# A linear-attention, routed-expert and gated-layer kernel: the attention stage laid out over 128 partitions, two batches at a time, with loads on two queues

## Chip, core and metric

The kernel runs on one core of a Trainium2 chip. Its five engines are TensorE (PE in the profile, its weight loads apart as PEld), VectorE (DVE), ScalarE (ACT), GpSimd (POOL) and SyncE (SP). The metric is the device time of one execution, in microseconds (us); lower is better.

## What is computed

Three layers follow each other. The first one, attention without a softmax, is where most of the change lies.

```python
def _attn_ref(q, k, v, g_norm):                  # each 8 x 8 x 576 x 64 (batch, head, token, width)
    kv = np.einsum('bhsd,bhse->bhde', k, v)
    out = np.einsum('bhsd,bhde->bhse', q, kv)
    rms = np.sqrt(np.mean(out * out, axis=-1, keepdims=True) + 1e-06)
    return (out / rms * g_norm)

def _moe_ref(x, modality_id, w_gate, modality_bias, w1, w2):   # x: 4608 x 512, 8 experts, F = 1024
    logits = x @ w_gate + modality_bias[modality_id]
    e_idx = np.argmax(logits, axis=1)
    ...
    for e in range(E):
        mask = e_idx == e
        h = np.maximum(x[mask] @ w1[e], 0.0)
        out[mask] = gate_w[mask, None] * (h @ w2[e])

def _moe2_ref(x, w_gate, w_val, w_out):           # 512 -> 1536 -> 512
    gate = 1.0 / (1.0 + np.exp(-(x @ w_gate)))
    val = x @ w_val
    return (gate * val @ w_out)
```

All inputs are float32.

## The kernel before

The program has four stages: attention, routing, expert tiles, gated layer. Each engine runs its own stream of instructions, and the streams meet only in semaphores (`wait_ge`, `then_inc`).

**Attention.** A batch's 576 tokens lie on R = 96 partitions, J = 6 tokens on each. So one partition's run in a load of q, k or v is 6 x 64 floats, 1536 bytes for each head, and a batch's load of one of the three is 1152 KB. SyncE issues all loads, one queue, double-buffered by batch (L384, L385, L387). One *step* handles one of the six tokens of each partition, for all eight heads, so there are 48 steps (8 batches of 6). Work of different steps overlaps: `At(i, s, lag)` says which step an operation serves. In a step

- ScalarE gathers the step's q out of `qt` into `qp` (L550); TensorE transposes it, four transposes (L926); ScalarE copies the result to `qT` (L530);
- TensorE multiplies `qT` by `kvx`, four matmuls (L911), one per pair of heads. `kvx` holds, for each pair, the two 64 x 64 products of k and v and 16 further columns, which are those products times the router's weights, so the router's logits come out of the same matmul. The outputs stand in one of two places in PSUM (`pair_outs`), so the matmuls of step n wait for the last reader of step n - 2 (`lgh_made`);
- ScalarE squares (L517), VectorE sums (L714), ScalarE takes the root (L512), VectorE the reciprocal (L692), VectorE normalises the outputs into `xn` (L704) and the router's columns into `lgh` (L708), and adds these up over heads into `logits` (L696) a step later;
- GpSimd multiplies `xn` by `g_norm` into `xb` (L457). SyncE stores `xb` to HBM once a batch is complete.

In four of the six steps TensorE also computes the k-v products of the batch, 12 matmuls of 96 rows by 64 columns a step (L942). In the other two it makes the router's columns: ScalarE copies the products to `kvx` (L539), TensorE transposes (L950), ScalarE copies to `kvT` (L544), TensorE multiplies by the router's weights (L918), ScalarE copies (L524). These chores are spread over the steps.

During attention, SyncE also loads the first expert's eight weight units (512 KB each, into the two buffers `raw`), behind the batches' loads, and VectorE splits them in each step into a high and a low part (L673, L679), since the expert matmuls work with float32r high parts and low remainders.

**Routing.** Once all logits are there, VectorE picks experts, counts and makes one-hot tables (L728 to L773, most on arrays of 96 x 384). 48 matmuls, one per step column, turn these into the token tables (L962), which VectorE reads (L784). GpSimd then gathers the first tile of tokens (L477).

**Experts and gated layer.** Tiles of 128 tokens, gathered by expert, pass two matmuls each; the next expert's weights are loaded into `raw` and split by VectorE meanwhile. Then come nine blocks of 512 tokens through the gated layer, bound by TensorE (L1047, L1058).

## Time and profile before

| | us |
|---|---|
| median of 3 runs | 1633.44 |
| fastest, slowest run | 1631.88, 1639.65 |
| span of the profiled execution | 1628.0 |
| TensorE busy in that span | 1547.1 (95%) |
| mean granted TensorE clock | 0.978 of full |

The profile gives the profiled execution its span, from first to last instruction; what a timed run has around the span is the difference, 5.4 us to the median. A granted clock of 1.00 in the rows is 2.4 GHz, 0.50 is 1.2 GHz. "DMA share" is how busy the core's 16 DMA engines were on average; it can read a little over 1 since a packet's record spans its overlap with the next.

### The profile page before, as it was taken

The numbers are of one execution on the slowest core, as the hardware profiler recorded it, in microseconds if no ns is written. First come the engines' busy times: TensorE is split into PE (matmuls) and PEld (weight loads), VectorE is DVE, ScalarE is ACT, GpSimd is POOL, SyncE is SP. The second block draws the span as 40 slices with busy tenths as digits, with TensorE's granted clock in tenths as the row PEclk, the third lists the DMA queues.
The fourth block names the chain that finished last, engine by engine and source line by source line (L and its number), as shares of the span: only waits on it lengthen the run. The fifth ranks groups of instructions, "written<-read, shape, count | busy, mean of one in ns | idle before, by whom it ended". The sixth has DMA issues, their size and how long they took to land.

```text
span 1628.0 us, 23019 instructions
## 1 busy us (share of the span) xinstructions
PE 1547.1 (95%) x7924; PEld 1297.4 (80%) x7925; DVE 559.8 (34%) x938; ACT 397.9 (24%) x744; POOL 181.3 (11%) x298
## 2 busy tenths in 40 slices
PE   6988479999999999969999999999999999999998
PEld 5878368888888888858888888888888888888886
DVE  2877743364524552233312212122121221212111
ACT  2766112222222222233221211112111121111111
POOL 1443122222222222100000000000000000000000
PEclk9999589999999999989999999999999999999999
DMA  9998223243314332043110000101001010010000
GB/s 226 257 266 232 81 75 106 71 154 129 120 47 136 112 128 64 31 134 103 65 52 1 30 23 1 53 1 52 1 1 52 1 52 1 0 52 0 27 0 26
DMA packets 56321, 120.61 MB, mean 74 GB/s; under 512 B 7614, under 2 KB 32190, under 8 KB 55488
## 3 DMA queue, kind: packets, MB, share of 16 engines
q1 hardware_dynamic: 49856, 99.75, 20.9%
q0 software_dynamic: 6400, 19.93, 4.0%
q8 instruction: 49, 0.80, 0.2%
q14 instruction: 16, 0.13, 0.0%
HBM read 91.33 MB, written 29.38 MB: 74 GB/s over the span
## 4 chain that ended last, share of the span: by engine, by line
PE 58%; issue 25%; DMA 6%; POOL 4%; POOLq 3%; DVE 1%; SPq 1%; ACT 0%; DVEq 0%; ACTq 0%
PE ps L1047 36%; PE ps L1058 18%; DMA vt<-in_v 4%; POOL xg L477 3%; POOLq L476 2%; PE ps L942 1%; PE ps L911 1%; PE ps L1037 1%; DMA raw<-in_moe_w 1%; POOL hold L471 1%; POOL from_now L475 1%; POOLq L484 0%; DMA x_rows<-xb 0%; DVE ssum L714 0%; POOL y_rows L485 0%
## 5 line engine op out<-in xcount | busy, mean ns | idle before, releaser
L1047 PE MATMUL ps<-yhi,gv 128*128 128x512 f32 x1728 | 548.1, 389 | 1.5 <-DVE ylo L874 1.5
L1047 PEld LDWEIGHTS ps<-yhi,gv 128*128 128x128 f32 x1728 | 324.3, 188 | 69.2 <-issue 1.9
L1047 PE MATMUL ps<-ylo,gv 128*128 128x512 f32 x864 | 336.1, 389 | 0.0
L1058 PE MATMUL ps<-wo,shi 128*128 128x512 f32 x864 | 266.9, 390 | 1.4 <-DVE slo L892 1.4
L890 DVE TENSOR_TENSOR s<-ps,sig 128x512 f32<-128x512 f32 x108 | 74.7, 692 | 489.2 <-ACT sig L609 489.2
L992 PE MATMUL ps<-ew,xhi 128*128 x640 | 203.3, 399 | 2.2 <-DVE xlo L811 1.7
L1014 PE MATMUL ps<-ew,hhi 128*128 x640 | 197.2, 389 | 1.3 <-DVE hlo L822 1.3
L1058 PEld LDWEIGHTS ps<-wo,shi 128*128 128x128 f32 x864 | 161.5, 188 | 35.0 <-DVE slo L892 1.9
L1047 PEld LDWEIGHTS ps<-ylo,gv 128*128 128x128 f32 x864 | 162.2, 188 | 33.7
L609 ACT ACTIVATE sig<-ps 128x512 f32<-128x512 f32 x108 | 64.7, 599 | 500.5 <-PE ps L1047 500.5
L1058 PE MATMUL ps<-wo,slo 128*128 128x512 f32 x432 | 168.2, 389 | 0.0
L892 DVE TENSOR_TENSOR slo<-s,shi 128x512 fp32r<-128x512 f32 x108 | 74.8, 692 | 204.4 <-ACT shi L612 204.4
L1014 PEld LDWEIGHTS ps<-ew,hhi 128*128 128x128 f32 x640 | 120.1, 188 | 26.4 <-issue 1.5
L992 PEld LDWEIGHTS ps<-ew,xhi 128*128 128x128 f32 x640 | 118.2, 190 | 26.0 <-issue 3.1
L992 PE MATMUL ps<-ew,xlo 128*128 x320 | 126.0, 394 | 0.0
L1014 PE MATMUL ps<-ew,hlo 128*128 x320 | 124.8, 390 | 0.0
L612 ACT CAST shi<-s 128x512 fp32r<-128x512 f32 x108 | 67.5, 625 | 215.5 <-PE ps L1058 208.0
L816 DVE COPY y<-ps 128x512 f32<-128x512 f32 x40 | 27.7, 691 | 219.4 <-PE ps L1014 219.4
L679 DVE TENSOR_TENSOR ew<-raw,ew 128x1024 f32 (+2 forms) x88 | 97.0, 1102 | 8.1
L1058 PEld LDWEIGHTS ps<-wo,slo 128*128 128x128 f32 x432 | 81.1, 188 | 17.0
L573 ACT CAST hhi<-ps 128x512 fp32r<-128x512 f32 x80 | 43.1, 590 | 208.6 <-PE ps L1001 208.6
L568 ACT ACTIVATE h<-ps 128x512 f32<-128x512 f32 x80 | 48.0, 600 | 164.3 <-PE ps L992 164.3
(139 smaller groups left out, 1280.0 us busy)
## 6 DMA issues: line engine op xcount, KB each, us to landing
raw<-in_moe_w SPq DMA_DIRECT2D x64, 512.0 KB, 4.0
qt<-in_q SPq DMA_DIRECT2D x8, 1152.0 KB, 13.3
x_rows<-xb SPq DMA_DIRECT2D x8, 1152.0 KB, 15.0
yin<-y_rows SPq DMA_DIRECT2D x18, 512.0 KB, 5.5
out<-ot SPq DMA_DIRECT2D x18, 512.0 KB, 2.9
kt<-in_k SPq DMA_DIRECT2D x7, 1152.0 KB, 20.2
vt<-in_v SPq DMA_DIRECT2D x7, 1152.0 KB, 25.1
graw<-in_moe_w_gate SPq DMA_DIRECT2D x6, 512.0 KB, 3.6
```

Source lines behind the costliest of these rows:

```text
L477: nc.gpsimd.indirect_dma_start(out=xg[:, t.p], out_offset=None, in_=x_rows, in_offset=bass.IndirectOffsetOnAxis(ap=from_now[:, t.p:t.p + 1 ...
L568: nc.scalar.activation(h[:, 512 * f:512 * f + 512], ps[:, 1 + f, :], ACT.Relu).then_inc(h_made, 1)
L573: nc.scalar.copy(hhi[:, 512 * f:512 * f + 512], ps[:, 3 + f, :]).then_inc(hhi_made, 1)
L609: nc.scalar.activation(sig[:], ps[:, 2 * (f % 2), :], ACT.Sigmoid).then_inc(sig_made, 1)
L612: nc.scalar.copy(shi[:], s32[:]).then_inc(shi_made, 1)
L679: made = nc.vector.tensor_tensor(lo_part, raw[:, u, cols], hi_part.bitcast(F32), ALU.subtract)
L890: nc.vector.tensor_tensor(s32[:], ps[:, 2 * (f % 2) + 1, :], sig[:], ALU.mult).then_inc(s_made, 1)
L892: nc.vector.tensor_tensor(slo[:], s32[:], shi[:].bitcast(F32), ALU.subtract).then_inc(slo_made, 1)
L992: last = mm(ps[:, 1 + f, :], x[:, t.p, rows], weights(e, c, part, cols), start=first, stop=end)
L1014: last = mm(ps[:, 5, :], x[:, rows], weights(e, DC + c // 2, part, cols), start=first, stop=end)
L1047: last = mm(ps[:, 2 * (f % 2) + part, :], gv[f // 2][:, w, part, d, cols], x[c % 2][:, d, :], start=first, stop=end)
L1058: last = mm(ps[:, 4 + m, :], s[:, rows], wo[f // 2][:, w, f % 2], start=(f == 0 and s is shi and w == 0), stop=(f == GC - 1 and s is slo))
```

## The change

**Layout.** The tokens of *two* batches now share the 128 partitions: batch 2g on partitions 0 to 63, batch 2g + 1 on 64 to 127, with J = 9 tokens on each partition. There are G = 4 such groups and 36 steps in place of 48. A partition's run in a load is 9 x 64 floats, 2304 bytes per head.

**Loads.** k and v come in halves of four heads, with three slots, q in two. The half of a load that goes to partitions 0 to 63 is issued by SyncE, the other by ScalarE (`load_half`, `load_q`, `load_next`). ScalarE's stand in `kv_keep`, between the copy of the products and the copy of their transpose.

**TensorE.** The k-v products are made of matmuls with 64 rows and 64 columns, a quarter of the array each (two row halves for the batches, two column halves for the heads of a pair), 72 in a row for each half of the heads (`kv_of`). The output matmuls use all rows and 64 columns, one for each batch, eight a step instead of four (`out_of`). The loop over steps is written out; the products of the next group stand in two lumps, one ahead of step 7's outputs and one behind the last outputs, and the router's columns (`chain_of`) behind that.

**Around it.** `g_norm` is no longer multiplied into x: it is multiplied into w1 when the weights are split (`g_tab`, a scalar operand per partition). VectorE writes `xb` directly. GpSimd, which did that product, now gathers q into `qp` and stores `xb` in pieces of three steps (12 a kernel, 6144 bytes per partition, instead of 8 of 12288). Half of the copies of the products move from ScalarE to VectorE. The first expert's weights are loaded in one go after the last k and v, into a place where those stood (`raw0`). ScalarE makes their high parts after attention, VectorE their low parts while TensorE makes the token tables.

```diff
-    R = 96
-    J = SEQ // R
-    T = BATCH * J
+    HALF = 64
+    R = 2 * HALF
+    J = SEQ // HALF
+    G = BATCH // 2
+    T = G * J
...
+        def load_half(engine, m, b):
+            g, heads = m // 2, slice(HH * (m % 2), HH * (m % 2) + HH)
+            rows = slice(HALF * b, HALF * b + HALF)
+            engine.dma_start(kt[rows, m % SLOTS], k_v[g, b, :, heads]).then_inc(k_in[m % SLOTS], 16)
+            engine.dma_start(vt[rows, m % SLOTS], v_v[g, b, :, heads]).then_inc(v_in[m % SLOTS], 16)
+        def load_next(engine, g, b):
+            if 2 * g + 3 < 2 * G:
+                engine.wait_ge(pe_kv, 2 * g + 1)
+                load_half(engine, 2 * g + 3, b)
+            if g + 1 < G:
+                wait(engine, qp_made, J * g)
+                load_q(engine, g + 1, b)
+            if 2 * g + 4 < 2 * G:
+                engine.wait_ge(pe_kv, 2 * g + 2)
+                load_half(engine, 2 * g + 4, b)
...
         @block.sync
+            for g in range(G):
+                load_next(sp, g, 0)
+            sp.wait_ge(pe_kv, 2 * G)
+            for c in range(DC):
+                sp.dma_start(raw0[:, c], w1_v[0, c]).then_inc(raw_in[c % 2], 16)
...
         @block.gpsimd
+            def qp_of(n):
...
+                nc.gpsimd.tensor_copy(qp[:, n % 3].rearrange("p (h d) -> p h d", h=HEADS),
+                                      qt[:, g % 2, :, DH * j:DH * j + DH]).then_inc(qp_made, 1)
+            def store_x(c):
...
+                nc.gpsimd.dma_start(x_v[g, :, at:at + STORE], xb[:, c % XSLOTS]).then_inc(x_out[c % XSLOTS], 16)
...
         @block.scalar
+            def kv_keep(g):
...
+                    nc.scalar.copy(kvx[half, g % 2, 0, :, DH * n:DH * n + DH],
+                                   ps[half, 0, 0:PAIRS * DH].rearrange("p (h d) -> p h d", h=PAIRS)).then_inc(kv_kept[0], 1)
+                load_next(act, g, 1)
+                wait(act, pe_m[0], g)
+                act.wait_ge(pe_kvt[0], g + 1)
+                nc.scalar.copy(kvT[:, 0].rearrange("p h d -> p (h d)"), ps[:, 0, :]).then_inc(kvt_kept[0], 1)
...
+            def first_high(u):
+                act.wait_ge(raw_in[u % 2], 16 * UNITS // 2)
+                nc.scalar.activation(ew[:, u, 0], raw0[:, u], ACT.Copy, scale=g_tab[:, u // 2:u // 2 + 1]).then_inc(w_high, 1)
...
         @block.vector
-                    made = nc.vector.tensor_tensor(lo_part, raw[:, u, cols], hi_part.bitcast(F32), ALU.subtract)
+                    made = nc.vector.scalar_tensor_tensor(out=lo_part, in0=raw[:, u, cols], scalar=scale, in1=hi_part.bitcast(F32),
+                                                          op0=ALU.mult, op1=ALU.subtract)
...
         @block.tensor
-                    for n in range(2):
-                        for j in range(J):
-                            cols = slice(DH * j, DH * j + DH)
-                            last = mm(ps[DH * n:DH * n + DH, 0, DH * a.j:DH * a.j + DH], kt[:, a.bp, 2 * a.j + n, cols],
-                                      vt[:, a.bp, 2 * a.j + n, cols], start=(j == 0), stop=(j == J - 1))
+            def kv_of(m):
...
+                for hp in range(PAIRS // 2):
+                    at = DH * (PAIRS // 2 * (m % 2) + hp)
+                    for j in range(J):
+                        cols = slice(DH * j, DH * j + DH)
+                        for b in range(2):
+                            rows = slice(HALF * b, HALF * b + HALF)
+                            for n in range(2):
+                                last = mm(ps[DH * n:DH * n + DH, b, at:at + DH], kt[rows, s, 2 * hp + n, cols],
+                                          vt[rows, s, 2 * hp + n, cols], start=(j == 0), stop=(j == J - 1))
+                last.then_inc(pe_kv, 1)
+            def out_of(n):
...
+                for hp in range(PAIRS):
+                    for b in range(2):
+                        rows = slice(HALF * b, HALF * b + HALF)
+                        last = mm(pair_outs(n % 2)[rows, hp, 0:KX], qT[:, n % 3, hp, rows], kvx[:, g % 2, b, hp, :], start=True, stop=True)
```

The first place is TensorE in the middle of attention, before the change: each step has outputs (L911), transposes (L926) and a small portion of k-v products (L942). The shapes are those of the output.

```order
L911 MATMUL ps<-kvx,qT 96x144 x4
L924 REGISTER_ALU
L926 MATMUL ps<-ident,qp 128x96 x4
L942 MATMUL ps<-vt,kt 64x64 x12
L911 MATMUL ps<-kvx,qT 96x144 x4
L924 REGISTER_ALU
L926 MATMUL ps<-ident,qp 128x96 x4
```

And after the change, at the end of a group: outputs are L973, transposes L981, products L945, the router's columns L954 and L959.

```order
L973 MATMUL ps<-kvx,qT 64x144 x8
L981 MATMUL ps<-ident,qp 128x128 x4
L945 MATMUL ps<-vt,kt 64x64 x72
L973 MATMUL ps<-kvx,qT 64x144 x8
L981 MATMUL ps<-ident,qp 128x128 x4
L973 MATMUL ps<-kvx,qT 64x144 x16
L945 MATMUL ps<-vt,kt 64x64 x72
L954 MATMUL ps<-ident,kvx 128x128 x8
L959 MATMUL ps<-gwg,kvT 128x8 x8
```

The products have moved out of the steps into two lumps of 72, the second of them, with the router's columns, between the groups.

The second place is ScalarE at a batch's chores, before the change: copy of the products (L539), gather of q (L550), root (L512), square (L517), copy of the transposed q (L530), copy of the transposed products (L544).

```order
L539 COPY kvx<-ps 64x4x64 x2
L550 COPY qp<-qt 96x512
L512 ACTIVATE rms<-ssum,eps 96x8
L517 ACTIVATE sq<-ps 96x512
L530 COPY qT<-ps 128x384
L544 COPY kvT<-ps 128x512
```

And after the change, where one group ends and the next begins: the same copies are L497, L502 and L506, and L277, L278, L281 issue loads.

```order
L512 ACTIVATE rms<-ssum,eps 128x8
L497 COPY kvx<-ps 64x4x64 x2
L277 DMA kt<-in_k 64x4x576
L278 DMA vt<-in_v 64x4x576
L281 DMA qt<-in_q 64x8x576
L277 DMA kt<-in_k 64x4x576
L278 DMA vt<-in_v 64x4x576
L502 COPY kvT<-ps 128x512
L506 COPY kvx<-ps 64x4x8 x2
```

Five load issues now stand on ScalarE's own stream between two links of the chain that readies the next group, and no step's work is interleaved with it.

## Rows read from the trace of the kernel before

**Rows 1.** Busy time by stage, all engines; then clock, DMA share, GB/s.

```profile
0.00:30.20 30.20, 15.49 (x128) 14.44 (x129) 6.51 (x19) 7.57 (x16) 1.91 (x10) 1.00 1.02 219
30.20:176.10 145.90, 126.02 (x1312) 114.99 (x1312) 113.00 (x283) 92.49 (x219) 59.88 (x48) 0.95 0.94 236
...
213.20:1628.00 1414.80, 1392.74 (x6428) 1158.75 (x6428) 415.73 (x577) 296.59 (x507) 114.59 (x232) 0.99 0.16 54
```

**Rows 2.** Chain that ended last, in time: start, length, what.

```profile
59.19 25.47 DMA vt<-in_v
...
97.04 25.70 DMA vt<-in_v
```

**Rows 3.** Windows of `xb`'s instructions: length, POOL busy, clock, DMA share, GB/s.

```profile
30.00:66.00 36.00, 14.02 (x11) 1.00 1.09 245
66.00:69.00 3.00, 1.27 (x1) 1.00 1.01 413
...
90.00:100.00 10.00, 4.74 (x4) 1.00 1.10 222
```

**Rows 4.** Timeline, one step late in attention: start, length, instruction, idle before.

```profile
166.85 0.49 PE L926 MATMUL ps<-ident,qp 96*128 96x96 f32 x4
...
168.32 1.22 PE L911 MATMUL ps<-kvx,qT 128*96 128x144 f32 x8 [0.97 <-DVE lgh L708]
...
169.64 0.59 ACT L517 ACTIVATE sq<-ps 96x512 f32<-96x512 f32 x1 [0.38 <-PE ps L911]
...
170.71 0.67 DVE L714 TENSOR_REDUCE ssum<-sq 96x8 f32<-96x512 f32 x1
...
171.48 0.30 ACT L512 ACTIVATE rms<-ssum,eps 96x8 f32<-96x8 f32 x1 [1.25 <-DVE ssum L714]
172.21 0.19 DVE L692 RECIPROCAL rstd<-rms 96x8 f32<-96x8 f32 x1
...
172.50 0.69 DVE L704 TENSOR_TENSOR xn<-ps,rstd 96x512 f32<-96x512 f32 x1
173.11 0.21 DVE L708 TENSOR_TENSOR lgh<-ps,rstd 96x64 f32<-96x64 f32 x1
...
173.27 1.26 POOL L457 TENSOR_TENSOR xb<-xn,g_row 96x512 f32<-96x512 f32 x1 [1.26 <-DVE xn L704]
```

**Rows 5.** Timeline of TensorE, one step's k-v products (24 records, 12 matmuls).

```profile
65.73 1.43 PE L942 MATMUL ps<-vt,kt 96*64 96x64 f32 x24
```

**Rows 6.** Windows of L942 inside that step: PE busy (records), PEld busy (records).

```profile
66.33:66.43 0.10, 0.10 (x9) 0.10 (x8) 1.00 1.22 492
66.53:67.15 0.62, 0.62 (x14) 0.50 (x9) 1.00 1.11 440
```

**Rows 7.** Timeline: a batch's chores, from products to router's columns.

```profile
75.74 0.76 ACT L539 COPY kvx<-ps 64x256 f32<-64x256 f32 x2 [0.67 <-PE ps L942]
...
78.28 0.59 ACT L544 COPY kvT<-ps 128x512 f32<-128x512 f32 x1
...
79.61 0.95 PE L918 MATMUL ps<-gwg,kvT 128*128 128x8 f32 x8
```

**Rows 8.** Timeline of SyncE's queue: how long an issue held it.

```profile
8.68 0.54 SPq L384 DMA_DIRECT2D kt<-in_k  x1
...
11.17 5.88 SPq L387 DMA_DIRECT2D qt<-in_q  x1
```

**Rows 9.** Timeline: end of attention, routing; last a split of a whole unit.

```profile
176.53 1.43 DVE L679 TENSOR_TENSOR ew<-raw,ew 128x256 fp32r<-128x256 f32 x1
...
186.28 0.55 DVE L762 TENSOR_TENSOR r_pos<-r_scan,r_off 96x384 f32<-96x384 f32 x1
...
192.55 3.55 DVE L773 TENSOR_TENSOR r_low<-col_t,r_lo 96x1536 bf16<-96x1536 int16 x4
193.55 10.75 PE L962 MATMUL ps<-r_hv,r_low 96*128 96x88 bf16 x48 [8.92 <-DVE r_low L773]
...
226.20 1.23 DVE L679 TENSOR_TENSOR ew<-raw,ew 128x1024 f32 x1
```

More of the change, by code:

```diff
@@ new lines, in qt_keep @@
+            def qt_keep(n):
+                wait(act, pe_out, n - 2)
+                act.wait_ge(pe_qt, n + 1)
+                nc.scalar.copy(qT[:, n % 3], ps[:, 2 + n % 2, :].rearrange("p (h r) -> p h r", h=PAIRS)).then_inc(qt_kept, 1)
+            kv_keep(0)
+            for g in range(G):
+                for i in range(PIPE):
+                    if i >= LAG_NORM:
+                        rms_of(J * g + i - LAG_NORM)
+                    if LAG_OUT <= i < J + LAG_OUT:
+                        sq_of(J * g + i - LAG_OUT)
+                    if i < J:
+                        qt_keep(J * g + i)
+                if g + 1 < G:
+                    kv_keep(g + 1)
@@ new lines, in _ @@
+            kv_keep(0)
+            for g in range(G):
+                for i in range(PIPE):
+                    n = J * g + i - LAG_NORM
+                    if i >= LAG_NORM:
+                        rstd_of(n)
+                        norm_of(n)
+                    if LAG_OUT <= i < J + LAG_OUT:
+                        ssum_of(n + 1)
+                    if i >= LAG_NORM and n % STORE == STORE - 1:
+                        logits_of(n // STORE)
+                if g + 1 < G:
+                    kv_keep(g + 1)
@@ L781, in _ @@
                 one_hot(r_low, r_lo, 128, n, 1).then_inc(hot_made, 1)
+            for u in range(UNITS):
+                dve.wait_ge(w_high, u + 1)
+                nc.vector.scalar_tensor_tensor(out=ew[:, u, 1], in0=raw0[:, u], scalar=g_tab[:, u // 2:u // 2 + 1], in1=ew[:, u, 0].bitcast(F32),
+                                               op0=ALU.mult, op1=ALU.subtract).then_inc(w_split, 1)
             dve.wait_ge(pe_table, 1)
@@ new lines, in chain_of @@
+            def chain_of(g):
+                for b in range(2):
+                    pe.wait_ge(kv_kept[b], 2 * (g + 1))
+                    for hp in range(PAIRS):
+                        last = nc.tensor.transpose(ps[:, b, 128 * hp:128 * hp + 128], kvx[:, g % 2, b, hp, 0:128], ident[:])
+                    last.then_inc(pe_kvt[b], 1)
+                for b in range(2):
+                    pe.wait_ge(kvt_kept[b], g + 1)
+                    for hp in range(PAIRS):
+                        last = mm(ps[:, b, E * hp:E * hp + E], kvT[:, b, hp, :], gwg[:, hp, :], start=True, stop=True)
+                    last.then_inc(pe_m[b], 1)
@@ new lines, in out_of @@
+            def out_of(n):
+                g = n // J
+                if n % J == 0:
+                    for b in range(2):
+                        pe.wait_ge(m_kept[b], 2 * (g + 1))
+                wait(pe, lgh_made, n - 1)
+                pe.wait_ge(qt_kept, n + 1)
+                for hp in range(PAIRS):
+                    for b in range(2):
+                        rows = slice(HALF * b, HALF * b + HALF)
+                        last = mm(pair_outs(n % 2)[rows, hp, 0:KX], qT[:, n % 3, hp, rows], kvx[:, g % 2, b, hp, :], start=True, stop=True)
+                last.then_inc(pe_out, 1)
@@ new lines, in qt_of @@
+            def qt_of(n):
+                wait(pe, qt_kept, n - 1)
+                pe.wait_ge(qp_made, n + 1)
+                for hp in range(PAIRS):
+                    last = nc.tensor.transpose(ps[:, 2 + n % 2, 128 * hp:128 * hp + 128], qp[:, n % 3, 128 * hp:128 * hp + 128], ident[:])
+                last.then_inc(pe_qt, 1)
+            kv_of(0)
+            kv_of(1)
+            pe.wait_ge(const_made, 6)
+            chain_of(0)
+            for g in range(G):
+                for i in range(J + LAG_OUT):
+                    if i >= LAG_OUT:
+                        out_of(J * g + i - LAG_OUT)
+                    if i < J:
+                        qt_of(J * g + i)
+                    if i == J - 2 and g + 1 < G:
+                        kv_of(2 * g + 2)
+                if g + 1 < G:
+                    kv_of(2 * g + 3)
+                    chain_of(g + 1)
```

360 lines of the change are left out of this document (144 added, 216 removed).

## The prediction

> **What bounds the kernel now.** I read the busy times by stage first [rows 1]. After 213.2 us TensorE is busy 1392.7 of 1414.8 us, and the change leaves that part's matmuls alone; what can be won lies before it. Attention runs to 176.1 us, 145.9 us of it with all four compute engines working and none full (TensorE 126.0, VectorE 113.0), while the DMA engines' share is 0.94. The chain of waits says which of these ends last: it twice runs for 25 us along a load of v [rows 2]. So I looked at what the loads get. While loads alone run, the DMA engines are full (share 1.09, 1.10) and move 245 and 222 GB/s; in a stretch with a store and weights among them, they move 413 at share 1.01 [rows 3]. Loads of q, k and v are slow for the engines' time that they take. Their volume is 24 x 1152 KB = 28.3 MB, which at 240 GB/s is 118 us; stores (9.4 MB) and first weights (4.2 MB) at 413 GB/s add 33. That is 151 us, to which the last batch's compute comes: attention is bound by loads, with compute close behind.
>
> **A step after the change.** Its closed loop goes over two steps, as the outputs have two places: outputs, square, sums, root, reciprocal, normalise, gates. By the rows 1.22 + 0.59 + 0.67 + 0.30 + 0.19 + 0.69 + 0.21 = 3.87 us [rows 4], and seven hand-overs of some 0.07 us (the outputs end at 169.54, the square starts at 169.64) make 4.35, so 2.15 us a step. Lengths on 128 partitions are those on 96, since elements per partition stay. VectorE loses the split portions from its steps and GpSimd's product; its own 1.76 us of work fits in 2.15. GpSimd's gather of q is not in the trace: below it lies a ScalarE pass over as many elements (the square, 0.59), above it GpSimd's product of that size, 1.26 us [rows 4]; either fits in 2.15, so it costs nothing.
>
> This stands on the eight output matmuls taking as long as the four did, that is on two column halves working at once. The trace has such matmuls: the two heads of a pair in L942 use the two column halves, one after the other. A step's 24 records take 1.43 us, about 58 ns each [rows 5]. In the last 0.62 us 14 records show. With a record of length d every 58 ns, 14 = (0.62 + d) / 0.058, so d is 0.2 us. In the 0.10 us where the heads change, 9 show; (0.10 + 0.2) / 9 is 33 ns [rows 6]. At that place nearly two run at a time, and the weight loads bunch too (8 records). So tiles do overlap, for as far as the queue reaches the other tile's matmuls. After the change neighbours in the program are always different tiles.
>
> Against this speaks a rule of the Trainium skill ("TensorE: Matmul & The Clock Gate", Part 3, The mechanism): a weight load overlaps running matmuls only when it goes to other rows. The two halves of an output use the same rows, so by that rule they would take turns, which is the last rival below. The bunched weight loads are of one row group, so the row goes against the rule, and I follow the row.
>
> **A lump of products**, 72 matmuls or 144 records: one at a time 144 x 0.058 = 8.4 us, two at a time 4.2, four at a time 2.1. I take 4.2, as the row shows two and never more; both ends stay.
>
> **A group.** Eight spacings of 2.15 = 17.2. The first lump, 4.2, less the free time of two steps' TensorE (2.15 - 1.22 - 0.5 each) = 3.3. The last outputs 1.2, the second lump 4.2. Then nothing else can run: copies of the products 0.76, transposes hidden under five load issues on ScalarE, 5 x 0.54 = 2.7 [rows 8], copy 0.59, router's columns for the first batch 0.95 [rows 7], and for the second 0.5 of the same (its copy was ready, and a first matmul's latency is in the row), copies 0.4, hand-overs 0.5: 6.4. Sum 32.3 us. The two small copies and the share of the second batch are my estimates, half a microsecond each way.
>
> **Loads.** A group is 7.08 MB of loads and 2.36 MB of stores. Rate of the loads: not in the trace for 2304-byte runs on two queues. Below, 240 GB/s as now; above, the 413 of the mixed stretch. I take 300, nearer to the slow rows since most of the traffic is of the same kind. Then a group needs 23.6 + 5.7 = 29.3 us, under its 32.3: compute binds, narrowly. The first outputs need 7.08 MB, 23.6 us, plus 3 until data flow and 2.4 of gather, transposes and copy: they start at 29.
>
> **End of attention.** 29 + 3 x 32.3 + last group (17.2 + 1.2 + 3.1 from square to gates; no lump in it) = 147.4, against 176.1 [rows 1]: 28.7 us less.
>
> **Routing.** The last split portions, 1.43 us ahead of the first routing operation, are gone. Arrays of 384 columns become 288: 0.55 to about 0.45 for each of a dozen, 1.5 us in all with the scan. One-hot tables shrink by a quarter; of the 7.3 us from `r_pos` to the first table matmul they are some 4.5 by my estimate, so 1.1 us. TensorE's 48 table matmuls in 10.75 us become 36 in 8.1. VectorE meanwhile has the tables' rest, 2.0 us, and now eight low parts, 8 x 1.23 = 9.8 [rows 9]; so it is VectorE that ends last, 11.8 us after the matmuls' start, 1.1 later than TensorE did. Sum: -1.4 - 1.5 - 1.1 + 1.1 = -2.9 us. The low parts have cover for 6.1 of their 9.8 us; without it routing would end later than before. ScalarE's eight high parts (about 1.1 each, as twice a 0.59 copy) begin with its last root; two stand ahead of the exponential, which VectorE asks for some 3 us later. The first weights, 4.2 MB behind the last k and v, at 300 to 413 GB/s take 10 to 14 us and are there by 137, before attention ends.
>
> **Experts and gated layer.** Same matmuls. The splits take a scalar per partition and the low part a three-operand instruction; if each high part went up to the low part's 1.23 us, VectorE would do 56 x 0.54 = 30 us more in a stage where it is busy 29%. I count nothing, at most 3 us.
>
> **Sum.** The profiled span of 1628.0 becomes 1628.0 - 28.7 - 2.9 = 1596.4. The median of the runs stands 5.4 above the span, so 1602.
>
> **Rivals.**
> - *Four tiles at a time.* Lumps 2.1, outputs 1.0: a group's compute is 16.6 + 1.2 + 1.0 + 2.1 + 6.4 = 27.3 (the step is 2.08 with outputs of 1.0), and loads at 300 bind at 29.3. End 28 + 3 x 29.3 + 21 = 137, 1591; with faster loads 131, 1585. For it speaks that 9 records in 0.10 us leave room to read more; against it that the trace never shows three tiles.
> - *Loads stay at 240 GB/s.* Then a group takes 29.5 + 5.7 = 35.2, the last q is there at 3 + 118 + 14 (stores before it) = 135, and the end is 135 + 2.4 + 21.5 = 159 to 164: 1612 to 1617. For it: the present rate at full share; a run of 2304 bytes is not much longer than 1536, and each load reaches only 64 partitions. The Trainium skill ("DMA: Bandwidth & Descriptors", Issuing engines are not separate DMA queues) says that a second issuing engine saves only issue time. By that rule the second queue gives no rate and this rival stands; no row here has two load queues. Against it: full engines moved 413 GB/s from 66 to 69 us, in the midst of a load of v [rows 2, 3].
> - *ScalarE stuck on its own issues.* One load held SyncE's queue for 5.88 us while three or more stood before it [rows 8]. SyncE has nothing else to do; on ScalarE the transpose's copy is behind it, and behind that TensorE. With 5 us more in each of three groups: 1611 to 1616. Against it: at a group's end most of ScalarE's earlier loads have landed.
> - *Tiles take turns* (the other side). Then outputs take 2 x 1.15 = 2.3, a step is TensorE's 2.3 + 0.5 = 2.8, lumps 8.4: a group is 22.4 + 8.4 + 2.3 + 8.4 + 6.4 = 48, the end 30 + 144 + 28 = 202, and the time 1633 + 26 - 4 = 1655. It decides from a group length of 43 us (29 + 3 x 43 + 21.5 = 179.5, where routing's gain is used up). Lumps in turns but outputs at once give 41 and 1627, about no change. Against it stand the bunched records.
>
> **Chances.** Forecast 0.50 (1592 to 1610), four at a time 0.15, loads at 240 0.14, ScalarE stuck 0.09, turns 0.12, half of it outputs too. The range of 1583 to 1627 leaves out the turns of the outputs and what is beyond the fast end. Within 0.5%, 8 us, is about what a measurement of this kernel can't tell from no change: 1625 to 1642. Faster 0.87, same 0.06, slower 0.07.
>
> **What would show it.** In the changed profile: first outputs near 29 us; their starts 2.15 apart inside a group, eight instructions (16 records) in about 1.2 us; a lump of 144 records in about 4.2 us; 12 to 13 us from a group's last outputs to the next group's first; GB/s near 300 and a DMA share under 1 in places; last normalise near 147; VectorE, not TensorE, ending the token tables, and first expert matmuls near 180. Wrong it would be if lumps took 8 us, if ScalarE's issues ran to several us, or if groups waited for q.

## The result and the profile after

The changed kernel takes 1646.07 us (median of 5 runs, 1643.68 to 1648.23), against 1633.44: 1.0061 of before, 95% interval 1.0039 to 1.0082. It is slower, by 0.6%, where 1602 was forecast. The profiled execution took 1648.23 us, its span is 1645.6. In each of the changed kernel's runs the time stands 2.6 to 2.7 us above the span, and some 1.8 us in each later run of before; so the 5.4 us between span and median of before, ahead of the prediction, are mostly a profiled execution that was some 3.6 us faster than the median.

The stages of the changed kernel, as windows (length; busy time and records of TensorE, its weight loads, VectorE, ScalarE, GpSimd; clock, DMA share, GB/s): start and attention, experts, gated layer.

```profile
0.00:30.20 30.20, 4.12 (x144) 3.97 (x145) 3.57 (x10) 1.49 (x2) 2.86 (x10) 0.84 0.97 213
30.20:182.70 152.50, 110.65 (x1824) 92.30 (x1824) 74.06 (x181) 60.28 (x130) 27.75 (x47) 0.80 0.84 230
218.80:714.20 495.40, 492.16 (x2396) 411.67 (x2396) 214.77 (x270) 111.88 (x201) 114.63 (x229) 1.00 0.30 100
729.80:1640.10 910.30, 908.86 (x4016) 744.99 (x4016) 198.72 (x295) 177.03 (x295) 0.00 (x0) 1.00 0.07 26
```

The same windows of before, for the last two stages:

```profile
213.20:708.20 495.00, 492.92 (x2396) 412.31 (x2396) 208.30 (x270) 111.55 (x201) 113.28 (x229) 0.99 0.31 100
724.90:1622.50 897.60, 896.12 (x4016) 743.14 (x4016) 198.71 (x295) 177.70 (x296) 0.00 (x0) 1.00 0.08 26
```

Two things went otherwise than forecast. Attention ends at 182.7 instead of 147.4 ([rows 1]: 176.1 before). And the gated layer, where the same 4016 records run, takes 12.7 us longer with TensorE full in both kernels. Routing and what lies between the stages give back 2.1 us.

The 12.7 us have two parts. One is the clock at the start of the layer. TensorE has little work for some 10 us ahead of it, and the granted clock is at 0.50 there. Before, it is back at 1.00 when the layer begins; in the changed kernel it is still low for most of the first 5 us, and 14 records start where 22 did, which is 8 x 0.227 = 1.8 us. First the changed kernel, then before:

```profile
729.80:734.80 5.00, 5.00 (x14) 3.98 (x15) 3.50 (x3) 2.40 (x3) 0.00 (x0) 0.61 0.00 0
724.90:729.90 5.00, 4.99 (x22) 4.17 (x23) 3.50 (x3) 2.96 (x3) 0.00 (x0) 1.00 0.01 3
```

The other part, 11 us, is spread evenly over the layer; the first experiments are about it.

The start of attention in the chain of waits (start, length, what; SPq and ACTq are issues of loads):

```profile
6.74 4.64 SPq L277
11.42 24.96 DMA vt<-in_v
36.52 4.15 PE ps L945 x144
41.45 0.54 ACTq L278
...
43.40 4.45 ACTq L278
47.89 0.59 ACT kvT L502
48.53 3.58 PE ps L959 x16
52.11 1.80 PE ps L981 x8
53.91 2.12 PE ps L973 x16
```

SyncE's half of the second v is there at 36.5; only then the second lump (72 products, 144 records) runs, and 17 us of chain come behind it. And the end of the first group, from the same chain:

```profile
65.69 1.20 PE ps L973 x16
...
67.48 2.26 PE ps L945 x144
69.74 1.12 PE ps L973 x14
70.86 1.44 issue
...
76.93 1.44 PE ps L945 x88
78.38 3.82 issue
...
84.02 0.37 ACT kvx L497
...
84.78 0.76 ACTq L278
...
87.54 0.84 ACTq L278
...
89.12 3.58 PE ps L959 x16
92.70 1.80 PE ps L981 x8
```

A lump takes 2.26 us and a step's outputs 1.20. That is 15.7 ns a record in the lump, against 58 where tiles come one after the other ([rows 5]), so nearly four tiles work at once. But twice TensorE stands in the midst of its own stream with nothing to wait for ("issue"), 1.44 and 3.82 us, ScalarE's issues stand between its copies, and the router's products take 3.58 us.

### The profile page after: what moved, and what is told of

The parts are those of the page before. It is cut to its first block, busy times and chain, and to the rows that moved or that the text cites. A ratio compares the mean times of both kernels' runs of the same rounds, so it can differ in the third digit from the quotient of the medians.

```text
span 1645.6 us, 23593 instructions
## 1 busy us (share of the span) xinstructions
PE 1527.9 (93%) x8440; PEld 1263.1 (77%) x8441; DVE 530.7 (32%) x835; ACT 368.1 (22%) x648; POOL 150.3 (9%) x298
## 4 chain that ended last, share of the span: by engine, by line
PE 59%; issue 26%; POOL 4%; POOLq 3%; DVE 2%; DMA 2%; ACT 1%; ACTq 1%; SPq 1%; DVEq 0%
PE ps L1092 36%; PE ps L1103 18%; POOL xg L455 3%; POOLq L454 2%; DMA vt<-in_v 2%; PE ps L973 1%; PE ps L1082 1%; PE ps L945 1%; DVE xb L712 1%; DVE ssum L728 1%; PE ps L959 1%; PE ps L981 1%; POOL hold L449 1%; ACTq L278 0%; POOLq L462 0%
## 5 line engine op out<-in xcount | busy, mean ns | idle before, releaser
L1103 PE MATMUL ps<-wo,shi 128*128 128x512 f32 x864 | 272.5, 396 | 1.4 <-DVE slo L918 1.4
L671 DVE SCALAR_TENSOR_TENSOR ew<-raw,g_tab,ew 128x1024 f32 x56 | 72.0, 1286 | 8.3 <-DVE ew L665 4.4
```

Of the source, the lines that this page charges most:

```text
L671: made = nc.vector.scalar_tensor_tensor(out=lo_part, in0=raw[:, u, cols], scalar=scale, in1=hi_part.bitcast(F32), op0=ALU.mult, op1=ALU.su ...
L1103: last = mm(ps[:, 4 + m, :], s[:, rows], wo[f // 2][:, w, f % 2], start=(f == 0 and s is shi and w == 0), stop=(f == GC - 1 and s is slo))
```

## The experiments

"Last gates" is the start of the last `lgh` instruction; "first" that of the first outputs; "gated" the length of the gated layer. Ratios are against before, run on the same chip. Before itself and the changed kernel stand on top for comparison.

| kernel | median us | ratio, interval | first | last gates | gated |
|---|---|---|---|---|---|
| before | 1633.44 | | 25.2 | 175.9 | 897 |
| changed | 1646.07 | 1.0061, 1.0039 to 1.0082 | 53.8 | 182.5 | 910 |
| before_shift | 1649.06 | 1.0101, 1.0072 to 1.0130 | 25.0 | 180.7 | 908 |
| shift_64 | 1639.73 | 1.0041, 1.0023 to 1.0059 | 24.3 | 182.6 | 903 |
| shift_256 | 1633.48 | 1.0006, 0.9983 to 1.0030 | 24.7 | 180.7 | 897 |
| shift_all | 1636.06 | 1.0030, 1.0008 to 1.0051 | 24.3 | 181.4 | 897 |
| after_align | 1635.02 | 1.0008, 0.9991 to 1.0025 | 52.6 | 179.0 | 899 |
| before_unrolled | 1635.32 | 1.0005, 0.9982 to 1.0028 | 24.9 | 181.2 | 899 |
| act_later | 1640.19 | 1.0019, 0.9998 to 1.0041 | 50.5 | 183.3 | 899 |
| one_queue | 1630.95 | 0.9983, 0.9964 to 1.0001 | 41.2 | 176.0 | 899 |
| spread1 | 1641.16 | 1.0046, 1.0023 to 1.0069 | 52.6 | 186.3 | 899 |
| steady1 | 1631.57 | 0.9976, 0.9952 to 1.0001 | 53.5 | 178.6 | 897 |
| two | 1631.93 | 0.9985, 0.9964 to 1.0006 | 43.6 | 173.9 | 899 |
| steady2 | 1619.08 | 0.9899, 0.9868 to 0.9929 | 47.8 | 165.1 | 897 |
| balanced | 1617.08 | 0.9898, 0.9866 to 0.9929 | 33.3 | 159.0 | 899 |
| steady3 | 1602.42 | 0.9823, 0.9798 to 0.9848 | 41.1 | 146.8 | 899 |
| steady4 | 1594.87 | 0.9757, 0.9726 to 0.9788 | 38.3 | 138.8 | 899 |
| merged, spread, steady | 2056, 2056, 2054 | 1.2567, 1.2566, 1.2552 | 145, 191, 191 | 599 to 602 | 897 to 899 |

One warning from this table: six kernels whose attention is that of before, or that of before written out, show last gates at 175.9, 180.7, 182.6, 180.7, 181.4 and 181.2. The profile of before is the earliest of them, so of attention's +6.6 us about 5 are the spread of single executions. On the whole time, the changed attention is level with the old one (after_align, 1.0008).

The last column has the clock of the layer's start in it as well. Every kernel with 899 us there has a granted clock of 0.57 to 0.71 in the layer's first 5 us, every one with 897 has 1.00; only before_unrolled has 899 at 1.00, and two stretches of 0.8 us without an instruction instead.

### Where the tiles lie

The change made the tiles ahead of the expert buffers 448 bytes larger. `ew`, `gv`, `wo`, `yhi`, `ylo` moved up by that; `sig`, `s32`, `shi`, `slo`, which lie below, did not.

```diff
+    shift = keep("shift", [128, 112], F32)      # before_shift
     raw = keep("raw", [128, 2, 1024], F32)
```

> The kernel before with one unused tile of 448 bytes put ahead of the expert buffers, so that every tile from there on (weights, transposed tokens, gated pieces) lies 448 bytes higher, as in the changed kernel, while the four small tiles of the gated layer stay where they are. Theory 'placement': the gated layer's output products start 231 or 236 ns apart instead of 227, a block of 512 tokens takes 100.9 us instead of 99.7, the layer 910 instead of 898 us, and the kernel 1645 us. Rival 'something else of the changed program' (its code's place, the clock, the state that attention leaves): 1633 us and 227 ns as before.

```diff
+    pad = keep("pad", [128, 16], F32)           # after_align
     raw = keep("raw", [128, 2, 1024], F32)
```

> The changed kernel with one unused tile of 64 bytes there, so that those tiles lie 512 bytes above where they lay before. Theory 'placement': the gated layer takes 898 us again and the kernel 1634 us, level with before. Rival: no change, 1646 us. If only the sum of both shifts counts and not their place within 128 or 512 bytes, it stays at 1646 too.

Both came as the theory said: the kernel before becomes 1.0% slower by an unused tile (14 us by the medians, 3 of them outside the gated layer), and the changed kernel becomes 11 us faster by another. In the gated layer the two pairs agree: 908.5 against 897.6 us at a clock of 1.00 from its start, 910.3 against 899.3 us with the slow start in both. TensorE's groups from 900 to 1500 us, first of before_shift, then of after_align (mean ns of one last; the first matmul row of each is gate and value, the others are the output):

```profile
L1048 PE MATMUL ps<-yhi,gv 128*128 128x512 f32 x1142 | 363.4, 390 | 0.0
L1059 PE MATMUL ps<-wo,shi 128*128 128x512 f32 x570 | 179.7, 396 | 0.0
L1059 PE MATMUL ps<-wo,slo 128*128 128x512 f32 x286 | 113.1, 395 | 0.0
```

```profile
L1093 PE MATMUL ps<-yhi,gv 128*128 128x512 f32 x1157 | 367.1, 389 | 0.0
L1104 PE MATMUL ps<-wo,shi 128*128 128x512 f32 x576 | 177.9, 390 | 0.0
L1104 PE MATMUL ps<-wo,slo 128*128 128x512 f32 x288 | 112.2, 389 | 0.0
```

The loss sits in the output products, whose weights are `shi` and `slo` and whose streamed columns are `wo`. The timeline of the changed kernel and of before, first and last of twelve of them and the next matmul:

```profile
1045.35 0.63 PE L1103 MATMUL ps<-wo,shi 128*128 128x512 f32 x2
...
1047.92 0.39 PE L1103 MATMUL ps<-wo,slo 128*128 128x512 f32 x1
1048.15 0.39 PE L1092 MATMUL ps<-yhi,gv 128*128 128x512 f32 x1
```

```profile
1035.00 0.62 PE L1058 MATMUL ps<-wo,shi 128*128 128x512 f32 x2
...
1037.49 0.39 PE L1058 MATMUL ps<-wo,slo 128*128 128x512 f32 x1
1037.72 0.39 PE L1047 MATMUL ps<-yhi,gv 128*128 128x512 f32 x1
```

Twelve take 2.80 us instead of 2.72, 233 ns a piece instead of 227, and the next six are late too (231 ns); 12 x 6.7 ns and 6 x 4 ns in each of 108 such rounds are 11 us. Which distance matters was then asked with other shifts of before:

> The kernel before with 64 unused bytes ahead of the expert buffers. Theory 'place within 128 bytes': slow as with 448 (which is 64 beyond a multiple of 128), products at 231 and 236 ns while the output products run, the gated layer 908 to 911 us, 1645 us. Rival 'the distance to the small tiles matters in larger steps (2 KB, 8 KB)': 1634.

> The kernel before with 256 unused bytes there. Theory 'place within 128 bytes': 897 us in the gated layer and 1634 us, as before. Rival 'place within 512 bytes' (the run with the 64 bytes on the changed kernel restored the place within 512 too): 1645.

> The kernel before with the 448 bytes put ahead of the small tiles as well, so that nothing moves against anything else in the gated layer. Theory 'relative place': 897 us in the gated layer, 1634 us, since what counts is where the weights loaded (s, 128 columns) lie against the columns streamed (w_out). Rival 'absolute place of the wide tiles': 909 us, 1646.

64 bytes cost about 3 us, far less than expected. The layer takes 903.5 us, but 2.9 of the 5.9 us over before are its slow start (33 records in the first 10 us, at clocks of 0.50 and 0.88, where before has 46). What is left agrees with the blocks behind it, 100.0 us each instead of 99.7. Only the products with `shi` are slower, 394 ns in their group against 390 in before, and 389 with `slo` in both. 256 and 512 bytes cost nothing in the layer, and 448 bytes under all tiles alike nothing (897.8 us; that kernel's whole time is still 0.3% over before, but not through this layer). So it is the distance between the small tiles and those above them, not the place of either, and the slower products are those that load weights from the one and stream columns from the other. Distances that differ from the old by 64 or 448 bytes cost, by 0, 256 and 512 don't. A rule with fewer words than that isn't shown by five points; why 64 spares `slo` stays open.

### What the loads get

> As the run with the 64 bytes, and every load of q, k and v issued by SyncE in the order of need (both batches of half 0, both of half 1, the constants, q, half 2, then as before), none by ScalarE. Theory 'order and holds': the second lump of products starts near 25 us instead of 36.5, since 4.7 MB at the 212 GB/s of the first 30 us are there by 23 us, ScalarE's holds of 6.2 us and 3.5 us between the copies fall away, first outputs near 38 instead of 53.8, attention ends near 163, and the kernel is 17 to 20 us under the run with the 64 bytes: near 1615. Rival 'a single queue carries less': the rate falls under 212 GB/s, the second lump starts no earlier than 33, and less than 8 us are won. Rival 'q and the later halves become late instead': groups get longer by what the start wins.

```diff
-            load_half(act, 0, 1)                # one_queue: and the other ACT loads
+            for b in range(2):
+                load_half(sp, 0, b)             # SyncE, both batches in turn
```

The second lump started at 26.9 instead of 35.4 and the first outputs came at 41.2 (38 forecast), but only 4 us of 17 to 20 were won: groups got longer, the third case named. The queues of this run and of the changed kernel (packets, MB, time as a share of 16 engines) say why. One queue alone, 30 to 40 us of one_queue; then the changed kernel, 50 to 60 us, where both queues happen to run:

```profile
DMA packets 978, 2.16 MB, mean 216 GB/s; under 512 B 47, under 2 KB 47, under 8 KB 977
q1 hardware_dynamic: 977, 2.14, 104.3%
```

```profile
DMA packets 1562, 3.47 MB, mean 347 GB/s; under 512 B 63, under 2 KB 63, under 8 KB 1561
q1 hardware_dynamic: 781, 1.73, 52.9%
q10 hardware_dynamic: 780, 1.72, 52.3%
```

The engines are full in both. A packet takes 1.043 x 160 / 977 = 0.171 us in the first and 0.529 x 160 / 781 = 0.108 us in the second. One queue writes to 64 partitions at a time; two write to both halves. I first tried to have one load reach all 128:

> As the single-queue run, but one load brings one head of both batches to all 128 partitions (64 rows and 64 rows of 2304 bytes), instead of one that brings four or eight heads of one batch to 64 partitions; the same packets, 96 loads instead of 40. Theory 'a load to 64 partitions uses half of the way in': packets of 2304 bytes take 93 to 115 ns instead of 175 to 180, as they do where both batches' loads happen to run together (111 ns at 50 to 60 us of the changed kernel), the rate with loads alone is 330 GB/s or more instead of 195 to 229, first outputs come near 32 us instead of 41.2, and the kernel takes 1605 to 1615. Rival 'the source's hops or the packet's size set it': 170 ns and more a packet, 1631 or, by the longer chain of issues (0.6 us each), more.

```diff
+                    engine.dma_start(tile[:, s, h], src[g, :, :, HH * (m % 2) + h])   # 2 x 64 x 576
```

It took 2056 us. Its queue from 20 to 30 us:

```profile
DMA packets 228, 0.52 MB, mean 52 GB/s; under 512 B 4, under 2 KB 4, under 8 KB 228
q1 hardware_dynamic: 228, 0.52, 13.0%
```

A share of 0.13 is that of two full engines of 16: the source's outermost dimension is the two batches, and by the share only two engines took part, each at 26 GB/s. The Trainium skill says so ("DMA: Bandwidth & Descriptors", Rules for kernel authors, use all 16 engines: an outermost dimension of size c confines a DMA to at most c engines), and the trace agrees. What it gives all the same is a packet's time with the way free: 0.130 x 160 / 228 = 0.091 us, so the 0.171 of a queue alone looks like nearly two engines behind each other.

Is it the second queue or the second half of the partitions that gives the rate? The changed kernel shows that one queue can do it. From 163 to 166.5 us SyncE's queue alone brings the first expert's weights, to all 128 partitions and mostly in packets of 2048 bytes:

```profile
DMA packets 712, 1.39 MB, mean 396 GB/s; under 512 B 45, under 2 KB 45, under 8 KB 712
q1 hardware_dynamic: 712, 1.39, 104.6%
```

That is 1.046 x 56 / 712 = 0.082 us a packet, half of what a packet of 2304 bytes takes where one queue writes to one half. No run has two queues writing to the same half. And the kernel before doesn't fit the rule: its loads reach 96 partitions and still got 222 to 245 GB/s ([rows 3]), which no run here explains.

Two more kernels built on the merged loads were bound by them; they bear on the stream of instructions alone, below:

> As the merged loads, and the products of the next group are made a few in each step (four heads' worth over five steps each) instead of in two lumps of 72. Theory 'instruction fetch starves the lumps': the stretches in which TensorE waits for nothing that the profile shows (21 us in all in the single-queue run, six of 1.8 to 5.1 us) go, since 256 instructions of one fetch now last 8 us and not 2; together with the last lump a group's chain is 5 to 8 us shorter, 15 us or more under the merged run. Rival 'fetches stand behind the loads wherever they are': the same total of such gaps, spread over the steps, and 2 to 5 us won by the last lump alone.

> As the spread run, but all 36 steps form one pipeline on every engine, the products of the next group fall in steps 0 to 5 of a group, its copies, transposes and logit products in steps 6 to 8. Theory: the gap between groups' outputs (12 to 17 us three times) falls to a step, so that the 36 steps take 36 x 2.15 = 77 us and some waits; with first outputs at 32 and 37.7 MB of loads and stores at 330 to 400 GB/s (95 to 114 us) attention ends at 112 to 125 us instead of 176 and the kernel takes 1570 to 1585. Rival 'the loads bind after all': at 245 GB/s 37.7 MB take 154 us, attention ends near 160, and the kernel takes about 1615.

In this layout, then, the two halves have to come from two queues at once, and evenly:

> The changed kernel with the 64 bytes and SyncE's loads of half 1 ahead of its eight small constants, so that both queues have the same order and neither batch's half runs ahead. Theory 'unequal queues': the second lump of products starts near 25 to 28 us instead of 35.4, and until then packets take 110 to 120 ns, since the two queues write to different partition halves at once; first outputs 8 to 10 us earlier, 1625 to 1628. Rival 'the order doesn't matter, the bytes do': no earlier than 33 us, 1634.

```diff
             load_half(sp, 0, 0)
+            load_half(sp, 1, 0)                 # ahead of the seven constants; was behind them
```

(The expectations say eight constants; seven loads stand there.) The second lump started at 18.6 us. It gave 9 us at the first outputs and 3 in the time, inside what the runs can tell. The constants still stood ahead of SyncE's q: from 20 to 30 us its queue moved 1319 small packets, 0.27 MB, while ScalarE's brought its half, and the two made 205 GB/s; TensorE then waited 6.1 us for the router's weights, which are made from the constants. The last step was to ask both halves together and the constants elsewhere:

> As the single pipeline with two queues, but ScalarE asks for its halves in the same steps as SyncE (half 3 and the second q ahead of its first copies, then in steps 3, 6 and 1), and the eight constants are asked by GpSimd. Theory 'drift between the queues': windows of 10 us with about 750 packets on each queue at 111 ns (as 50 to 60 us of the two-queue runs show) become the rule, the two waits of 15.7 and 12.9 us for the first batch's or second batch's v fall under 5 us each, the constants (31 us) no longer hold VectorE's first copies, and attention ends near 140 to 148 instead of 165: 1595 to 1603. Rival 'bytes': the waits stay and the time is within 5 us of 1619.

```diff
+            nc.gpsimd.dma_start(wg[:], ...)     # steady3: the constants, GpSimd
...
+                if i == 3 and 2 * g + 5 < 2 * G:
+                    act.wait_ge(pe_kv, 2 * g + 3)
+                    load_half(act, 2 * g + 5, 1)
```

Its queues from 20 to 30 us:

```profile
DMA packets 1756, 3.91 MB, mean 391 GB/s; under 512 B 64, under 2 KB 64, under 8 KB 1755
q10 hardware_dynamic: 877, 1.95, 52.4%
q1 hardware_dynamic: 878, 1.95, 52.3%
```

391 GB/s with loads of q, k and v alone, 0.095 us a packet. The Trainium skill ("SBUF — State Buffer", Door 1: The DMA port swizzle) says that partitions 0 to 63 reach 8 of the 16 ports into the buffers, and the trace agrees: 202 to 216 GB/s for one half. The Trainium skill goes on there that two loads to the two halves do not help ("Can I just issue two DMAs to hit both halves?", +6%); here they gave 391 against 216, and the measurement decides.

### The chain between groups, and the stream of instructions

> As the run with the 64 bytes, but ScalarE issues its share of the next loads behind its copies of kvT and m instead of between the copy of kv and that of kvT. Theory 'ScalarE is held by its own issues': the chain between two groups loses 6.2 us in front of the first outputs and 3.5 us in front of the second ones, so that the time falls by about 8 to 10 us, to 1626. Rival 'the loads bind': what the chain wins is waited for at the next half, whose load is asked 2 to 6 us later; the same time, 1635.

The first outputs came 2 us earlier, the last gates 4 later: what the chain won, the loads, asked later, took back. The rival held.

> The single pipeline over all 36 steps (products, copies, transposes and logit products of the next group inside the steps) with the single queue's loads to 64 partitions. Theory 'the loads bind at 64 partitions': two DMA engines write through one way into the buffers, so a packet of 2304 bytes takes twice the 93 ns that it took with two engines at work (merged run), 175 to 186 ns, and the loads end near 140 us whatever the order of the work; attention ends near 162 to 167, the kernel takes 1617 to 1622. Rival 'the chain between groups bound it': attention ends by 140, 1595.

As forecast by the theory on mechanism, 10 us off on size: with one queue even a single pipeline over all 36 steps wins nothing over groups (1631.6 against 1631.0). Its chain of waits runs for 28.9 us along one load of q.

> The single pipeline with two queues of equal order (SyncE brings the first batch of a pair, ScalarE the second, issued in its steps instead of between its copies). Theory: both halves are loaded together, packets at 110 to 120 ns, 300 to 330 GB/s; first outputs near 41 us, then 36 steps at 2.15 us where loads and stores (37.7 MB at 330 to 400 GB/s, 95 to 115 us) allow, no lumps, no chain between groups: attention ends at 120 to 130 us and the kernel takes 1578 to 1592. Rival 'ScalarE's holds': with the queue full it stands 3 to 6 us at each group's loads, inside the steps, 15 to 20 us more: 1600. Rival 'the loads bind at 205 to 245 GB/s all the same': as the steady single-queue run, 1617 to 1622.

```diff
-            for g in range(G):                  # steady1 to 3, on every engine
-                for i in range(PIPE):
+            for s in range(T + LAG_NORM):
+                g, i = s // J, s % J
```

1619, and not 1578 to 1592: ScalarE asked its half 13 us after SyncE's, and the queues ran alone by turns again. Steady3 put that right, and moved the constants to GpSimd with it. What of its gain is the pipeline's:

> The changed kernel with the 64 bytes, its groups and its two lumps of products, but with even queues: both queues in the same order, ScalarE's halves asked in its steps and never between its copies, the constants asked by GpSimd. Theory 'the rate was the first bound, the chain between groups the second': packets at 95 to 111 ns, first outputs near 41 us as in the last run, and then the groups' own length, 32 us forecast plus 4 to 8 us of waits for instructions: attention ends at 160 to 170, the kernel takes 1612 to 1622, half way between 1635 and 1602. Rival 'even queues are the whole gain': 1602 to 1606. Rival 'they give nothing without the pipeline': 1630 or more.

1617, as forecast: even queues with the groups and lumps of the changed kernel win 18 us (1635 to 1617), the pipeline on top 15 (to 1602). In the 18 us is also that ScalarE's issues no longer stand between its copies; the two weren't taken apart. The pipeline without the queues wins nothing. But balanced has its first outputs at 33.3, steady3 only at 41.1. The chain of steady3 shows why: it had ScalarE's issues of half 4 ahead of the copy of kvT again.

```profile
23.47 0.37 ACT kvx L508
23.84 0.39 ACTq L278
...
29.17 2.89 ACTq L279
...
32.10 0.59 ACT kvT L493
```

> As steady3, with ScalarE's issue of half 4 behind its copies of kvT and the router's columns instead of between the copies of kv and kvT, where it holds ScalarE for 8 us (4.94 and 2.89 us in the chain of waits). Theory 'ScalarE held by its issues counts once the loads have their rate': first outputs at 33 us as in the balanced run instead of 41.1, and attention ends 4 to 8 us earlier: 1594 to 1599. Rival 'the loads bind still, as in act_later': the later half 4 is waited for in the second group's products, and the time is within 2 us of 1602.

```diff
-            kv_keep(0, 0)
-            load_half(act, 4, 1)
-            for part in range(1, 3):
+            for part in range(3):
                 kv_keep(0, part)
+            load_half(act, 4, 1)
```

1594.87, the best kernel of the study: 2.4% under before (2.1 to 2.7), 51 us under the changed kernel, 11 of them the place of the tiles. The first outputs came 3 us earlier, not 8, but attention's end 8. Much the same move that gave nothing while the loads bound (act_later) gives 7.5 us once they have their rate.

> The kernel before with its attention loop written out for all eight batches instead of one loop of two batches. Theory 'instruction fetch': TensorE's stream shows stretches of 1 to 4 us in which it waits for nothing that the profile shows, as the changed kernel does (1.44, 3.82, 3.38 us), about one for each 200 or 300 products, and the queue that brings instructions moves 0.97 MB instead of 0.80. The time stays within 3 us of 1633 if loads cover them, 5 to 10 us more if they don't. Rival 'the gaps belong to the changed kernel's lumps of 144 products, which use up instructions fastest': no gap over 1 us here, 1633.

The rival held: its instruction queue moves twice as many packets in the first 220 us (12 against 6), but no such stretch in attention is over 0.4 us, and the time is that of before. Two of 0.8 us stand in its gated layer (at 1028 and 1229 us). The length of the program costs no more than that here.

> As the single-queue run (loads of 64 partitions, as there), and the products of the next group are made 16 at a time in the steps instead of in two lumps of 72. The merged runs could not tell this, since their loads came at 52 GB/s. Theory 'instruction fetch starves the lumps': the stretches of 1.8 to 5.1 us in which TensorE waits for nothing that the profile shows (21 us in the single-queue run) fall under 3 us in all. Whether that is seen in the time depends on the loads: at 205 GB/s alone q, k and v take 138 us and the stores of x 23 us more, so that 5 to 10 us are won at most: 1621 to 1628. Rival 'fetches stand behind the loads wherever they are': the gaps stay 15 us or more in all, 1631.

In the chain of waits of one_queue these stretches are 4.08, 5.06, 3.21, 4.65, 2.45 and 1.75 us; here 0.87, 3.40, 1.50, 2.60 and 2.01, so 10.4 us instead of 21.2. Half as much, not the 3 I expected, and the time rose by 10 us, since the products now stand ahead of outputs and wait there for their loads (32.1 us of waits for v, against 23.2). In the stretch from 78.38 of the changed kernel one packet of instructions came in (queue 8):

```profile
q1 hardware_dynamic: 339, 0.76, 100.1%
q8 instruction: 1, 0.02, 2.3%
```

That TensorE waits for its instructions there, behind loads that keep the engines full, is what the two runs and this row suggest. Merged, spread and steady fit it: with the engines 13% busy none of them has a stretch over 0.8 us, and merged's lumps of 144 records run through. But TensorE had waited over 33 us for data ahead of each of those lumps. The lumps themselves aren't needed: steady1, with 24 products in a step, has eight stretches of 1.15 to 3.63 us, 19.5 in all. No run takes the fetch itself away, so the cause is not shown.

## Why the prediction was wrong

By its own steps:

- **Tiles overlap: right, and more.** Steps start 2.15 us apart, as forecast (4.35 halved is 2.18, so the sum was read a little low). The lump was mis-sized on the safe side: 4.2 forecast, 2.26 measured (four tiles at a time, the first rival). The rule of the Trainium skill ("TensorE: Matmul & The Clock Gate", Part 3, The mechanism) that a weight load overlaps only with matmuls of other rows is not borne out: the eight output matmuls, two column halves of the same rows, take 1.20 us where the four took 1.22.
- **"I take 300" was the first failed step.** The range 240 to 413 missed what decides in this layout: whether both halves of the partitions are written at once. 202 to 216 GB/s where one queue runs, 347 to 391 where both do. In the changed kernel they take turns for much of the start, since seven constants (4.5 us of issues) stand ahead of SyncE's second half and none ahead of ScalarE's. The rival "loads stay at 240" had the sentence that each load reaches only 64 partitions and did not price it: below its lower end lay one queue's half rate.
- **"First outputs at 29": 53.84, the largest miss, 24.8 us.** 7.5 us lie ahead of the second lump, which starts at 36.5 on the last v. 17.3 us is chain that the step left out, as it took q for the last to come: lump 4.15 (clock 1.2 GHz after 19.5 us without work), ScalarE's issues 6.4, copies 1.0, router's products 3.6, transposes of q 1.8.
- **The group, 32.3: measured 40.7, 35.2, 30.7,** 9.7 us more in three. Its 6.4 us of chain left out q's transposes (1.8) and took the router's products at 1.45 where they are 3.5 to 3.6 (clock at 1.2 GHz again); stretches without instructions of 1.44, 3.82 and 3.38 us stand in no row of before. ScalarE's issues were 3.7 instead of 2.7. The short lumps gave some 3 us back.
- **Routing -2.9: measured -1.0.** VectorE's eight low parts end it, as said.
- **"Experts and gated layer: nothing" was the second failed step, 12.7 us.** It counted instructions and durations, and no row of before could show what a moved tile costs: 11.0 us. The other 1.7 are the clock, at 0.61 for the layer's first 5 us where it was 1.00. Without the moved tiles the change is level with before (after_align).
- **The last term, 5.4 us from span to median: measured 0.5** (1645.6 to 1646.07). The spans differ by 17.6 us, the medians by 12.6; the profiled execution of before was a fast one.

147.4 + 24.8 + 9.7 + 0.8 (last group 22.3 for 21.5) = 182.7, the measured end; with 1.9 in routing, 12.7 in the gated layer, 0.4 in the experts and -1.1 between the two, 1596.4 becomes the measured span, 1645.6. The rival "ScalarE stuck on its own issues" was in part right: the issues ran to 6.4 us before the first outputs, but moving them is worth something only behind faster loads (7.5 us in steady4, nothing in act_later). The forecast end of attention, 147.4, was reached by steady3 (147.0), with even queues and without groups; that its time is the forecast 1602 is chance, as it got there another way.

## What to carry to other kernels

Before splitting a load over partition groups, see that both halves of the partitions are written at the same time: one queue for each half, the same order, nothing small ahead on one of them, and issues on engines that aren't held. Check the queues' rows in windows of 10 us; shares that change places say that half the way in is idle. And when a change moves tiles, compare the mean length of the untouched matmuls first: a shift by 256 or 512 bytes cost nothing here, one by 64 bytes 3 us and one by 448 bytes 11 us, 0.7% of the kernel. Compare the granted clock at the start of each stage too before putting a difference down to the change.

## What the runs showed of the hardware

- Matmuls with 128 columns of weights and 512 streamed columns start 227 ns apart, or 231 to 236, by the distance in the buffers between the weights loaded and the columns streamed (before, shift_64, before_shift, shift_all; what differs between them is the distance between the tiles of the one and of the other).
- Matmuls of 64 rows and 64 columns on the four quarters overlap: 144 records in 2.26 us. At the lower clock level (1.2 GHz; 0.50 and 0.51 granted from 20 to 40 us, TensorE without work from 17.0 to 36.5) the same lump takes 4.15 us. The windows of the changed kernel, 20 to 40 us:

```profile
20.00:30.00 10.00, 0.00 (x0) 0.00 (x0) 0.42 (x2) 0.00 (x0) 0.00 (x0) 0.51 1.07 224
30.00:40.00 10.00, 3.48 (x131) 3.52 (x134) 2.02 (x7) 0.00 (x0) 0.00 (x0) 0.50 1.05 202
```

- A load whose source has the two batches outermost ran at the share of two engines, 52 GB/s.
- One queue moved 396 GB/s to 128 partitions and 216 GB/s to 64; two queues, one to each half, moved 391.
